# Retention in 64-token chunks with state and v stacked in K, the first layer run a block ahead, and weights split by layer

## The chip, the cores and the metric

The kernel runs on one core of a Trainium2 chip. The core has TensorE (PE) for matrix products, VectorE (DVE), ScalarE (ACT) and GpSimd (POOL) for elementwise work, and SyncE (SP), which here only starts transfers. The metric is the time of one execution on the device in microseconds (us), the median of several runs. Smaller is better. All arithmetic is in float32.

## The reference

Retention over 2 batches, 8 heads, 576 positions and head width 64 gives 1152 tokens of width 512. Four dense experts (512 to 1024 to 512, ReLU), weighted per token, follow; then one MLP (512 to 2048 to 512) with a mish-like activation.

```python
# retention
scores = (1 / sqrt(64)) * q @ k.T
Dmat = where(i >= j, gamma[h] ** (i - j), 0)
x = (scores * Dmat) @ v                     # then to [1152, 512]
# experts, e = 0..3
p = probs / (probs.sum(-1) + 1e-9)
out += p[:, e] * (relu(x @ w1[e]) @ w2[e])
# MLP
h = out @ w_in
y = (h * tanh(softplus(h))) @ w_out
```

## The kernel before, in words

**Retention.** The sequence of a batch is cut into 6 chunks of 96 tokens, 12 steps over both batches (loop `Fori(0, BATCH)`). For a step PE computes the masked scores of the next chunk (`scores`, L259, with q spread into a block-diagonal tile so that two heads share one product), the output from scores and v (L316), the output from the running state and q (L322), and the addition to the state k^T v (L296). ACT spreads q (L375) and copies the state out of PSUM (L387). DVE masks the scores (L480), scales the output with the decay of the rows (L510) and takes the low part of the split of x (L518). POOL scales v by the decay of the keys (L660).

**Splitting.** The large products use a fast format that keeps fewer bits, so each operand is kept as a high and a low part and each product is three matmuls: high by high (L265), high by low (L266), low by high (L267), each with 128 weights columns and 384 moving columns. ACT makes the high part of a weight (L186, `unit_hi`), POOL the low part (L191, `unit_lo`); for activations ACT makes `h_hi` (L416) and DVE `h_lo` (L525).

**Experts and MLP.** The MLP counts as two more "experts" of 1024 hidden columns. For each of 6 experts, 3 blocks of 384 tokens and 8 tiles of 128 hidden columns there are 12 matmuls of the first layer (`hidden`) and 12 of the second (`project`): 144 tiles, 3456 matmuls. The order on PE is written out by hand: the first layer of a tile is issued `AHEAD` = 3 tiles before its second layer. The hidden tiles go through a ring of `HR` = 4 PSUM banks, so a first layer also waits until the activation of four tiles earlier has been computed (`s_hf`). After each block DVE adds the four PSUM banks of the second layer to `acc_sb` (L546, L548). In the MLP each tile needs, one after the other, exp (ACT L438), `m_a` and `m_w` (DVE L596, L598), ln and exp (ACT L443, L445), `m_t` (POOL L686), `m_c`, `m_n`, `h_act` (DVE L605, L611, L614), then the split. Weights of an expert come in 8 units of 512 KB, each split in one operation of 128x1024 on ACT and one on POOL; the split of the next expert's units falls at the end of the last block of an expert and at the start of the next.

**Token weights.** DVE normalises the probabilities; ACT writes them to memory (`probs_by_expert<-p_norm`, L401), waits for that write (`s_ps`) at the last chunk of the first batch, and reads them back broadcast over the partitions (L407).

Of the kernel before, what the change touches and what calls it, by code (L numbers as in the profile page):

```python
# [19 lines left out]
CH = 96  # L36
CHUNKS = SEQ // CH
STEPS = BATCH * CHUNKS
PAIRS = HEADS // 2
MID = SEQ // 2  # L40
SLOTS = CHUNKS
# [6 lines left out]
TPE = PH * UNITS  # L48
KT = DM // P
UW = KT * P + DM  # L50
RAW = 4
HR = 4
AHEAD = 3
WARM = 9
LAG = 3

M0 = MOE_EXPERTS
# [3 lines left out]
def build(nc, qk_in, kv_in, row_decay_in, key_decay_in, mask_in, probs_in, weights_in, probs_dram, out_t):  # L62
    with ExitStack() as ctx:
# [3 lines left out]
        def sem(name):  # L67
            return ctx.enter_context(nc.semaphore(name))

        w_hi0 = sb("w_hi0", [P, RAW, UW], F32R)
        w_lo0 = sb("w_lo0", [P, RAW, UW], F32R)
        w_raw = sb("w_raw", [P, RAW, UW])
        x_hi = sb("x_hi", [P, KT, TOKENS], F32R)
        x_lo = sb("x_lo", [P, KT, TOKENS], F32R)
        acc_sb = sb("acc_sb", [P, KT, TOKENS])

        pb = sb("pb", [P, MOE_EXPERTS * TOKENS + TC])
# [9 lines left out]
        qk = sb("qk", [P, SLOTS, 2, PAIRS, CH], stack=attn)  # L89
        kv = sb("kv", [CH, SLOTS, 2, DM], stack=attn)  # L90
        row_decay = sb("row_decay", [P, CHUNKS, PAIRS, CH], stack=attn)
        key_decay = sb("key_decay", [CH, CHUNKS, HEADS], stack=attn)
        mask = sb("mask", [CH, CH], stack=attn)

        q_diag = sb("q_diag", [P, 2, PAIRS, 2, CH], stack=attn)
        s_masked = sb("s_masked", [CH, 2, PAIRS, 2, CH], stack=attn)

        state = sb("state", [P, 2, PAIRS, P], stack=attn)
# [3 lines left out]
        w_hi1 = sb("w_hi1", [P, UNITS - RAW, UW], F32R)  # L102
        w_lo1 = sb("w_lo1", [P, UNITS - RAW, UW], F32R)
        h_hi = sb("h_hi", [P, HR, TC], F32R)
        h_lo = sb("h_lo", [P, HR, TC], F32R)
        h_act = sb("h_act", [P, 2, TC])
# [7 lines left out]

        banks = [ctx.enter_context(nc.psum_tensor(f"bank{i}", [P, 512], F32)) for i in range(8)]

        HALF = PAIRS // 2
        ps_s = [[banks[2 * par + y][0:CH, 0:PAIRS * CH].rearrange("p (h x c) -> p h x c", h=HALF, x=2)
                 for y in range(2)] for par in range(2)]
        ps_state = banks[5][:, 0:PAIRS * DH].rearrange("p (h c) -> p h c", h=PAIRS)  # L120
        ps_o = [banks[6 + par][:, 0:PAIRS * CH].rearrange("p (h c) -> p h c", h=PAIRS) for par in range(2)]
        ps_acc = [banks[d][:, 0:TC] for d in range(KT)]
        ps_h = [banks[4 + i][:, 0:TC] for i in range(HR)]

        s_qk = [sem(f"s_qk{i}") for i in range(SLOTS)]
        s_kv = [sem(f"s_kv{i}") for i in range(SLOTS)]
        s_rowd = [sem(f"s_rowd{i}") for i in range(CHUNKS)]
        s_keyd = sem("s_keyd")
        s_mask = sem("s_mask")  # L130
        s_zs = sem("s_zs")
        s_qd = sem("s_qd")
# [3 lines left out]
        s_sm = sem("s_sm")  # L136
        s_o = sem("s_o")
        s_kvp = sem("s_kvp")
        s_st = sem("s_st")
# [6 lines left out]
        s_pb = sem("s_pb")  # L146
# [4 lines left out]
        s_g1 = sem("s_g1")  # L151
        s_acc = sem("s_acc")
        s_g2 = sem("s_g2")
# [51 lines left out]
        def _(sp):  # L205
# [547 lines left out]
```

## Time and profile before

| what | value |
|---|---|
| median of 3 runs | 688.27 us (685.68 to 689.82) |
| span of the profiled execution | 682.0 us |
| PE busy | 657.8 us (96%), 3993 matmuls |
| DVE busy | 362.5 us (53%) |
| ACT busy | 225.8 us (33%) |
| POOL busy | 187.2 us (27%) |
| memory traffic | 40.78 MB |

The span is the profiled execution from its first to its last instruction. No time of that execution as a whole is listed beside the span, so the 6.3 us between the span and the median of the runs are taken as what lies around the span. PE and PEld are the matmuls and the weight loads of TensorE; a matmul is pipelined with the next, so its own duration (some 337 ns) is longer than the distance to the next one. `L265` is line 265 of the kernel. The idle time in front of an instruction is named with what released it.

### The profile page before, as it was taken

Reading aid. Unit: us, or ns where it says so; the run is one execution under the profiler, and the core shown is the slowest. Engines: PE = TensorE matmul, PEld = TensorE weight load, DVE = VectorE, ACT = ScalarE, POOL = GpSimd, SP = SyncE. Lnnn points to the kernel's source line nnn. Section 1 sums busy time; section 2 is a strip of 40 time slices with the busy share of each in tenths; the row PEclk is TensorE's granted clock in tenths of the full one; section 3 lists DMA queues with packets and bytes.
Section 4 is the critical chain, followed back from the end, with each engine's and each line's share of the span. In section 5 each row is a group of like instructions: output and inputs, shape, how many; then the busy total and the mean of one; then the engine's idle time right before and its main releaser. Section 6 shows DMA issues by size and latency. Waiting matters only on the chain.

```text
span 682.0 us, 10838 instructions
## 1 busy us (share of the span) xinstructions
PE 657.8 (96%) x3993; PEld 643.8 (94%) x3993; DVE 362.5 (53%) x618; ACT 225.8 (33%) x405; POOL 187.2 (27%) x113
## 2 busy tenths in 40 slices
PE   8979999999999999999999999999899998799998
PEld 5868999999999999999999999999899997699997
DVE  5534532325232334232344242547997789988786
ACT  4554211133111133111133121235555454444442
POOL 2255400046000056000055000153423256532222
PEclk9989999999999999999999999999999999999999
DMA  9994300023000023000024000031100002001011
GB/s 276 293 281 167 123 1 1 1 93 124 31 0 0 0 92 134 20 0 0 0 93 153 0 0 0 0 122 63 62 0 0 0 31 92 0 0 46 0 46 46
DMA packets 13967, 40.78 MB, mean 60 GB/s; under 512 B 2304, under 2 KB 4608, under 8 KB 13952
## 3 DMA queue, kind: packets, MB, share of 16 engines
q1 hardware_dynamic: 12848, 38.22, 17.5%
q10 hardware_dynamic: 1104, 2.38, 1.1%
q8 instruction: 7, 0.11, 0.1%
q14 instruction: 8, 0.07, 0.0%
HBM read 38.22 MB, written 2.38 MB: 60 GB/s over the span
## 4 chain that ended last, share of the span: by engine, by line
PE 84%; DVE 7%; DMA 4%; ACT 2%; issue 2%; SPq 1%; DVEq 0%; ACTq 0%
PE bank L265 27%; PE bank L267 27%; PE bank L266 27%; DMA qk<-in_qk 4%; DVE m_a L596 3%; PE bank L259 1%; PE bank L322 1%; DVE m_c L605 1%; PE bank L316 1%; DVE m_w L598 1%; ACT m_u L438 1%; ACT w_hi L186 1%; DVE acc_sb L548 1%; ACT m_r L443 1%; DVE h_lo L525 1%
## 5 line engine op out<-in xcount | busy, mean ns | idle before, releaser
L265 PE MATMUL bank<-h_hi,w_hi 128*128 128x384 f32 x576 | 195.4, 339 | 12.9 <-DVE h_lo L525 11.3
L191 POOL TENSOR_TENSOR w_lo<-w_raw,w_hi 128x1024 fp32r<-128x1024 f32 x48 | 117.9, 2461 | 323.0 <-ACT w_hi L186 322.8
L266 PE MATMUL bank<-h_lo,w_hi 128*128 128x384 f32 x576 | 194.0, 337 | 0.0
L267 PE MATMUL bank<-h_hi,w_lo 128*128 128x384 f32 x576 | 194.0, 337 | 0.0
L267 PE MATMUL bank<-x_hi,w_lo 128*128 128x384 f32 x576 | 194.0, 337 | 0.0
L265 PE MATMUL bank<-x_hi,w_hi 128*128 128x384 f32 x576 | 193.7, 336 | 0.1
L266 PE MATMUL bank<-x_lo,w_hi 128*128 128x384 f32 x576 | 193.5, 336 | 0.0
L416 ACT ACTIVATE h_hi<-h_act 128x384 fp32r<-128x384 f32 x144 | 75.2, 522 | 290.2 <-DVE h_act L531 269.0
L531 DVE SCALAR_TENSOR_TENSOR h_act<-bank,pb 128x384 f32<-128x384 f32 x96 | 53.5, 557 | 178.8 <-PE bank L267 178.2
L525 DVE TENSOR_TENSOR h_lo<-h_act,h_hi 128x384 fp32r<-128x384 f32 x144 | 97.4, 676 | 67.2 <-ACT h_hi L416 67.2
L265 PEld LDWEIGHTS bank<-h_hi,w_hi 128*128 128x128 f32 x576 | 108.0, 187 | 16.9 <-DVE h_lo L525 13.8
L265 PEld LDWEIGHTS bank<-x_hi,w_hi 128*128 128x128 f32 x576 | 108.1, 188 | 0.3 <-issue 0.3
L266 PEld LDWEIGHTS bank<-x_lo,w_hi 128*128 128x128 f32 x576 | 108.2, 188 | 0.0
L266 PEld LDWEIGHTS bank<-h_lo,w_hi 128*128 128x128 f32 x576 | 108.1, 188 | 0.0
L267 PEld LDWEIGHTS bank<-x_hi,w_lo 128*128 128x128 f32 x576 | 108.1, 188 | 0.0
L267 PEld LDWEIGHTS bank<-h_hi,w_lo 128*128 128x128 f32 x576 | 108.0, 188 | 0.0
L686 POOL TENSOR_TENSOR m_t<-m_w,m_r 128x384 f32<-128x384 f32 x48 | 56.2, 1171 | 130.1 <-ACT m_r L445 130.1
L186 ACT ACTIVATE w_hi<-w_raw 128x1024 fp32r<-128x1024 f32 x48 | 50.7, 1056 | 34.3 <-PE bank L267 34.2
L596 DVE TENSOR_SCALAR m_a<-m_u 128x384 f32<-128x384 f32 x48 | 37.2, 775 | 29.8 <-ACT m_u L438 29.8
L443 ACT ACTIVATE m_r<-m_w 128x384 f32<-128x384 f32 x48 | 25.2, 526 | 46.6 <-DVE m_w L598 46.6
L438 ACT ACTIVATE m_u<-bank 128x384 f32<-128x384 f32 x48 | 23.3, 485 | 43.6 <-PE bank L267 43.6
L605 DVE SCALAR_TENSOR_TENSOR m_c<-m_r,m_t 128x384 f32<-128x384 f32 x48 | 30.7, 640 | 1.1 <-POOL m_t L686 0.3
(37 smaller groups left out, 321.3 us busy)
## 6 DMA issues: line engine op xcount, KB each, us to landing
w_raw<-in_weights SPq DMA_DIRECT2D x48, 512.0 KB, 3.3
qk<-in_qk SPq DMA_DIRECT2D x12, 384.0 KB, 13.3
kv<-in_kv SPq DMA_DIRECT2D x12, 384.0 KB, 14.6
pb<-probs_by_expert ACTq DMA_DIRECT2D x4, 576.0 KB, 8.9
out_t<-acc_sb SPq DMA_DIRECT2D x2, 768.0 KB, 3.6
row_decay<-in_row_decay SPq DMA_DIRECT2D x6, 192.0 KB, 7.6
out_t<-acc_sb SPq DMA_DIRECT2D x4, 192.0 KB, 1.9
mask<-in_mask SPq DMA_DIRECT2D x1, 36.0 KB, 3.7
```

The source lines that it names most:

```text
L186: act.activation(high(u), w_raw[:, u % RAW, :], ACT.Copy).then_inc(s_wh, 1)
L191: pool.tensor_tensor(low(u), w_raw[:, u % RAW, :], high(u).bitcast(F32), ALU.subtract).then_inc(s_wl, 1)
L265: pe.matmul(out, w[0], x[0], start=first, stop=False)
L266: pe.matmul(out, w[0], x[1], start=False, stop=False)
L267: return pe.matmul(out, w[1], x[0], start=False, stop=last)
L416: act.activation(h_hi[:, n % HR, :], h_act[:, n % 2, :], ACT.Copy).then_inc(s_hh, 1)
L443: act.activation(m_r[:, n % 2, :], m_w[:, n % 2, :], ACT.Ln, bias=2.0).then_inc(s_ln, 1)
L525: dve.tensor_tensor(h_lo[:, n % HR, :], h_act[:, n % 2, :], h_hi[:, n % HR, :].bitcast(F32), ALU.subtract).then_inc(s_hl, 1)
L531: dve.scalar_tensor_tensor(h_act[:, n % 2, :], ps_h[n % HR], 0.0, pb[:, bass.ds(e * TOKENS + (n // UNITS) * TC, TC)], ALU.max, ALU.mult).t ...
L596: dve.tensor_scalar(m_a[:, :], m_u[:, n % 2, :], MISH_CAP, 2.0, ALU.min, ALU.add).then_inc(s_ma, 1)
L605: dve.scalar_tensor_tensor(m_c[:, :], m_r[:, n % 2, :], 2.0, m_t[:, n % 2, :], ALU.mult, ALU.add).then_inc(s_mc, 1)
L686: pool.tensor_tensor(m_t[:, n % 2, :], m_w[:, n % 2, :], m_r[:, n % 2, :], ALU.mult)\
```

## The change

**Retention.** Chunks are of 64 tokens, 9 per batch, 18 in all. One tile `qkv` of 128 partitions holds a chunk: the lower 64 partitions ("keys") hold v and k by tokens, the upper 64 ("features") k and q by features. Scores of chunk c+1 read the upper half and write the lower half of PSUM; the state product of chunk c reads the lower half and writes the upper one; they alternate in PE's order (`scores_and_state`). ACT then copies the state over the k of the features half, and DVE writes the masked scores over the k of the keys half, so that `output` is one product of depth 128 per head, with v and the state stacked as weights and the masked scores and q stacked as moving operand. Spreading q (ACT L375), the state-by-q products (L322) and the two zeroed tiles go away. Row decays are made on DVE from a small constant tile in place of six loads.

**First layer ahead.** The first layer runs a block (8 tiles) ahead of the second, with `h_hi` and `h_lo` of 8 tiles each. The first 8 tiles of it are put in halves of 6 matmuls between the products of chunks 7 to 17. The PSUM ring of hidden tiles stays at 4.

**Weights.** A unit is split into two halves of 256 KB, one per layer; each is split by an operation of 128x512 (ACT, then POOL), spread over the blocks at 8 halves in 11 tiles by a table. There are 96 halves, of which 11 are split during retention.

**The MLP's second layer** has the tokens as weights columns and 512 moving columns of `w_hi`/`w_lo`: 9 matmuls of 128x512 for a tile in place of 12 of 128x384, into 3 PSUM banks, and the result is stored by tokens.

**Loops** are gone: every engine's program is written out, with constants in the waits. The read of the probabilities is issued on ACT at the start, the wait for `probs_by_expert` stands on ACT at chunk 2, and only 192 KB of the broadcast is read there.

```diff
-CH = 96
-CHUNKS = SEQ // CH
+CH = 64
+PER_BATCH = SEQ // CH
+CHUNKS = BATCH * PER_BATCH
...
+AFTER_SCORES = {7: (0, 0), 8: (1, 0), 9: (2, 0), 10: (3, 0), 11: (4, 0),
+                12: (5, 0), 13: (5, 1), 14: (6, 0), 15: (6, 1), 16: (7, 0), 17: (7, 1)}
+AFTER_OUTPUT = {7: (0, 1), 8: (1, 1), 9: (2, 1), 10: (3, 1), 11: (4, 1)}
...
+            def output(c):
...
+                for hp in range(PAIRS):
+                    for x in range(2):
+                        mm = pe.matmul(ps_o[DH * x:DH * (x + 1), hp], qkv[rows, c % SLOTS, 0, 2 * hp + x],
+                                       qkv[rows, c % SLOTS, 1, 2 * hp + x], start=True, stop=True)
...
+            for c in range(CHUNKS):
+                scores_and_state(c)
+                if c in AFTER_SCORES:
+                    hidden_half(*AFTER_SCORES[c])
+                output(c)
+                if c in AFTER_OUTPUT:
+                    hidden_half(*AFTER_OUTPUT[c])
+            for n in range(TILES):
+                if n + UNITS < TILES:
+                    hidden_ready(n + UNITS)
+                    hidden_products(n + UNITS, range(KT))
+                if n < MOE_TILES:
+                    project(n)
+                else:
+                    project_tokens(n)
...
+            def masked(c):
+
+                dve.wait_ge(s_sc, c + 1)
+                if has_state(c):
+                    dve.wait_ge(s_kv, states(c))
...
+                if c == 2:
+                    act.wait_ge(s_ps, 16)
+                    act.dma_start(pb[:, 0, 0:TC], probs_dram[0, 0:TC].partition_broadcast(P)).then_inc(s_pb0, 16)
```

How instructions stand on the engines: first PE in one step of the retention. Before, a step is state addition, scores of the next chunk, output from scores, output from the state (the names are PSUM banks, the tile of k and v, the spread q, the masked scores).

```order
L296 MATMUL bank<-kv 64x64 [waits s_st]
L296 MATMUL bank<-kv 64x64 x7
L255 REGISTER_ALU
L259 MATMUL bank<-q_diag,qk 96x192 [waits s_qd]
L259 MATMUL bank<-q_diag,qk 96x192 x3
L312 REGISTER_ALU
L316 MATMUL bank<-s_masked,kv 64x96 [waits s_sm]
L316 MATMUL bank<-s_masked,kv 64x96 x3
L316 MATMUL bank<-s_masked,kv 64x96 [waits s_sm]
L316 MATMUL bank<-s_masked,kv 64x96 x3
L322 MATMUL bank<-qk,state 128x96 x4
```

After, on PE at chunk 7: the last two of its 16 alternating score and state products, the first half of hidden tile 0, the 8 output products, and the start of that tile's second half.

```order
L268 MATMUL bank<-qkv 64x64
L272 MATMUL bank<-qkv 64x64
L314 MATMUL bank<-x_hi,w_hi 128x384 [waits s_wl,s_xl]
L315 MATMUL bank<-x_lo,w_hi 128x384
L316 MATMUL bank<-x_hi,w_lo 128x384
L314 MATMUL bank<-x_hi,w_hi 128x384
L315 MATMUL bank<-x_lo,w_hi 128x384
L316 MATMUL bank<-x_hi,w_lo 128x384
L308 MATMUL bank<-qkv 64x64 [waits s_st,s_xt,s_sm,s_vd]
L308 MATMUL bank<-qkv 64x64 x7
L314 MATMUL bank<-x_hi,w_hi 128x384
L315 MATMUL bank<-x_lo,w_hi 128x384
```

So the output products, which wait for the masked scores (`s_sm`), the copied state (`s_st`) and the row scaling of the chunk before (`s_xt`), stand right behind the scores and state products of the same chunk in chunks 0 to 6, and behind six first-layer matmuls from chunk 7 on.

ACT at the start of the changed kernel, from the state copy of chunk 0 to that of chunk 4:

```order
L409 ACTIVATE qkv<-bank 64x512 [waits s_kv,s_sc]
L445 DMA probs_by_expert<-p_norm 128x4x9 [waits s_pc]
L409 ACTIVATE qkv<-bank 64x512 [waits s_kv,s_sc]
L442 ACTIVATE x_hi<-x_tmp 128x4x64 [waits s_xt]
L409 ACTIVATE qkv<-bank 64x512 [waits s_kv,s_sc]
L442 ACTIVATE x_hi<-x_tmp 128x4x64 [waits s_xt]
L448 DMA pb<-probs_by_expert 128x384 [waits s_ps]
L409 ACTIVATE qkv<-bank 64x512 [waits s_kv,s_sc]
L442 ACTIVATE x_hi<-x_tmp 128x4x64 [waits s_xt]
L409 ACTIVATE qkv<-bank 64x512 [waits s_kv,s_sc]
```

The wait for the written probabilities (`s_ps`) has moved from the last chunk of the first batch to three state copies after the write is issued; the state copy of chunk 3 (the fourth L409 here) is queued behind it.

## Rows read from the trace of the kernel before

**Rows 1.** Page, parts 1 and 3: busy time by engine; instruction queues.

```profile
PE 657.8 (96%) x3993; PEld 643.8 (94%) x3993; DVE 362.5 (53%) x618; ACT 225.8 (33%) x405; POOL 187.2 (27%) x113
...
q8 instruction: 7, 0.11, 0.1%
```

**Rows 2.** Windows: start:end, length, busy us (instructions) by engine, PEclk, DMA share, GB/s.

```profile
10.00:20.00 10.00, 9.64 (x131) 8.26 (x130) 5.97 (x11) 5.70 (x13) 2.35 (x4) 1.00 1.05 306
...
36.00:40.00 4.00, 3.58 (x20) 2.87 (x22) 1.67 (x3) 2.59 (x5) 2.90 (x2) 0.57 1.03 270
...
100.00:450.00 350.00, 350.00 (x2003) 350.00 (x2002) 126.81 (x217) 75.66 (x118) 64.61 (x27) 1.00 0.11 39
450.00:500.00 50.00, 46.57 (x264) 45.46 (x262) 40.35 (x59) 23.74 (x44) 22.55 (x14) 1.00 0.19 63
550.00:600.00 50.00, 41.30 (x227) 39.07 (x227) 44.53 (x59) 24.84 (x45) 29.36 (x18) 1.00 0.13 42
```

**Rows 3.** Chain that ended last, 0 to 70 us: start, length, what.

```profile
4.96 5.79 DMA qk<-in_qk
...
30.38 21.28 DMA qk<-in_qk
...
67.56 0.44 PE bank L265
```

**Rows 4.** The same chain, MoE stage: one matmul of three blocks.

```profile
120.82 0.18 PE bank L265
...
221.58 0.18 PE bank L265
```

**Rows 5.** The same chain, one step of retention on PE.

```profile
19.26 0.62 PE bank L296 x16
19.88 1.47 PE bank L259 x8
21.35 0.81 PE bank L316 x16
22.16 1.06 PE bank L322 x8
```

**Rows 6.** Timeline, start of the kernel: start, length, engine, line, operation.

```profile
0.74 0.40 SPq L207 DMA_DIRECT2D qk<-in_qk  x1
...
7.59 1.07 ACT L375 ACTIVATE q_diag<-qk 64x384 f32<-64x384 f32 x2 [2.34 <-DMA qk<-in_qk]
```

**Rows 7.** DMA view: issuing engine, count, KB each, median us from issue to landing.

```profile
p_nat<-in_probs SPq DMA_DIRECT2D x1, 18.0 KB, 3.3
probs_by_expert<-p_norm ACTq DMA_DIRECT2D x1, 18.0 KB, 11.7
```

**Rows 8.** Groups by line: count, busy us, mean ns, idle before and releaser.

```profile
L387 ACT ACTIVATE state<-bank 64x256 f32<-64x256 f32 x20 | 7.6, 378 | 0.8 <-issue 0.2
L438 ACT ACTIVATE m_u<-bank 128x384 f32<-128x384 f32 x48 | 23.3, 485 | 43.6 <-PE bank L267 43.6
L480 DVE TENSOR_TENSOR s_masked<-bank,mask 96x384 f32<-96x384 f32 x24 | 12.4, 546 | 5.4 <-PE bank L259 5.3
L548 DVE TENSOR_TENSOR acc_sb<-bank,acc_sb 128x384 f32<-128x384 f32 x48 | 23.5, 549 | 0.9 <-PE bank L267 0.9
```

**Rows 9.** Timeline, PE after a wait in retention.

```profile
36.41 2.87 PE L259 MATMUL bank<-q_diag,qk 128*96 128x192 f32 x8 [2.28 <-ACT q_diag L375]
```

**Rows 10.** Timeline, MLP stage: DVE and POOL while weights are split.

```profile
565.70 2.39 POOL L191 TENSOR_TENSOR w_lo<-w_raw,w_hi 128x1024 fp32r<-128x1024 f32 x1
565.80 2.51 DVE L596 TENSOR_SCALAR m_a<-m_u 128x384 f32<-128x384 f32 x1 [0.34 <-ACT m_u L438]
571.37 2.38 DVE L596 TENSOR_SCALAR m_a<-m_u 128x384 f32<-128x384 f32 x1 [0.47 <-ACT m_u L438]
```

**Rows 11.** Timeline, MLP stage: DVE where no weights are split.

```profile
510.54 0.56 DVE L598 SCALAR_TENSOR_TENSOR m_w<-m_u,m_a 128x384 f32<-128x384 f32 x1
513.44 0.36 DVE L596 TENSOR_SCALAR m_a<-m_u 128x384 f32<-128x384 f32 x1 [0.22 <-ACT m_u L438]
513.84 0.56 DVE L598 SCALAR_TENSOR_TENSOR m_w<-m_u,m_a 128x384 f32<-128x384 f32 x1
```

**Rows 12.** Timeline, end: last matmul of PE.

```profile
678.68 0.34 PE L267 MATMUL bank<-h_hi,w_lo 128*128 128x384 f32 x1
```

**Rows 13.** Timeline, start of the second layer: PE's weight load.

```profile
67.55 0.19 PEld L265 LDWEIGHTS bank<-h_hi,w_hi 128*128 128x128 f32 x1 [1.05 <-issue]
```

More of the change, by code:

```diff
@@ new lines, in hidden_products, with hidden_half @@
+            def hidden_products(n, tiles):
+                c, t = n // UNITS % PH, n % UNITS
+                for k in tiles:
+                    at = slice(P * k, P * (k + 1))
+                    mm = three(ps_h[n % HR], (w_hi[:, 0, t, at], w_lo[:, 0, t, at]),
+                               (x_hi[:, k, cols(c)], x_lo[:, k, cols(c)]), k == 0, k == KT - 1)
+                if KT - 1 in tiles:
+                    mm.then_inc(s_g1, 1)
+            def hidden_half(t, half):
+                if half == 0:
+                    hidden_ready(t)
+                hidden_products(t, range(2 * half, 2 * half + 2))
@@ new lines, in project_tokens @@
+            def project_tokens(n):
+                g, t = n // UNITS, n % UNITS
+                if g % PH == 0:
+                    pe.wait_ge(s_wl, 2 * UNITS * (g // PH) + UNITS + t + 1)
+                pe.wait_ge(s_hl, n + 1)
+                for tt in range(TT):
+                    if t == 0:
+                        pe.wait_ge(s_af, emptied(g - 1, tt))
+                    rows = slice(P * tt, P * (tt + 1))
+                    mm = three(ps_out[tt], (h_hi[:, n % UNITS, rows], h_lo[:, n % UNITS, rows]),
+                               (w_hi[:, 1, t], w_lo[:, 1, t]), t == 0, t == UNITS - 1)
+                    if t == UNITS - 1 and tt < TT - 1:
+                        mm.then_inc(s_acc, 1)
+                mm.then_inc(s_g2, 1)
@@ L350, in _ @@
[L350 to L362 removed]
+            pe.wait_ge(s_slot[0], landed(0))
@@ new lines, in _ @@
+            for h in range(HEADS):
+                mm = scores_head(0, h)
+            mm.then_inc(s_sc, 1)
+            for c in range(CHUNKS):
[13 more added lines that the diff above has]
+                    project_tokens(n)
@@ L550, in add_up_from @@
-            def add_up_from(start, e, c):
-                with dve.If(e == start):
-                    add_up(e, c, first=True)
-                with dve.If(e > start):
-                    add_up(e, c)
-            def second_lo(c, tiles=range(KT)):
-                for d in tiles:
-                    dve.wait_ge(s_x2h, KT * c + d + 1)
-                    dve.tensor_tensor(x_lo[:, d, cols(c)], acc_sb[:, d, cols(c)],
-                                      x_hi[:, d, cols(c)].bitcast(F32), ALU.subtract)
```

836 lines of the change are left out of this document (381 added, 455 removed).

## The prediction, on record before the changed kernel ran

> **What bounds the kernel now.** I read the page first, then windows over the whole span, then the chain that ended last, and then timelines at the places where PE was not full. PE is busy 657.8 of 682.0 us [rows 1], and from 100 to 450 us it has no gap at all [rows 2]. There the kernel is a plain stream of matmuls. Its pace is read from the same place in blocks that are three apart: 221.58 - 120.82 = 100.76 us for 3 x 192 matmuls, 0.1749 us each [rows 4]. Of these, 160 ns are 384 columns at 2.4 GHz (granted clock 1.00) [rows 2]; 15 ns come on top.
>
> So the time of before divides into four pieces. Until 67.56 us runs the retention, with only 3 of the 144 first-layer tiles done; then the first second-layer matmul starts [rows 3]. The 3420 matmuls left take 3420 x 0.1749 = 598.3 us at that pace. The last matmul ends at 678.68 + 0.34 = 679.0 [rows 12], so 679.0 - 67.56 - 598.3 = 13.1 us are lost in between; 3.4 and 8.7 us of it are PE's idle time in 450 to 500 and 550 to 600 us [rows 2], both in the MLP, where DVE is busy 89% in the second. The last 3.0 us are the last addition and store.
>
> The retention is bound by input: transfers run at 306 GB/s with all 16 engines busy [rows 2], and the chain waits 5.8 and 21.3 us for q and k [rows 3]. One step costs PE 0.62 + 1.47 + 0.81 + 1.06 = 3.96 us [rows 5].
>
> **The change part by part.** *Retention on PE.* Each float32 product counts as two instructions. The nearest row for the new 64x64 products is L296, whose heads alternate between two halves of the output partitions: 16 in 0.62 us, 0.038 each [rows 5]. Scores and state together are 32 of them, 1.22 us; the output is 16, 0.61 us. That is 1.83 us for 64 tokens, 18 times 33 us, against 12 x 3.96 = 47.5 us. I take this, because scores and state alternate between disjoint halves too; the other bound is no overlap at all, 0.076 each.
>
> In chunks 0 to 6 nothing stands between the scores and the output. The output waits for the mask on DVE, which now also waits for the state product. L480 takes 0.546 us for 384 columns [rows 8], so 0.7 for 512; with 0.25 us of hand-over the chunk is 1.22 + 0.7 + 0.25 + 0.61 = 2.8 us. From chunk 7 on six first-layer matmuls (1.05 us) cover that chain, and they are work that would have to be done anyway.
>
> *Start.* Before, q of the second step was the seventh transfer, 1.45 MB in all, and was read at 7.59 us [rows 6]. Chunk 1 ends 1.27 MB (512 + 219 + 512 KB) after the same start, so about 7.0 us. Chunks 0 to 2 then end at 15.3, and the output of chunk 3 at 18.1.
>
> *The wait for the probabilities.* Their write took 11.7 us to land under full transfers, that of the read in the same state of the queues 3.3 [rows 7]. ACT issues it behind the state copy of chunk 0, which ends at 8.3 + 0.6 = 8.9 us (the copy by L387 and L438, 0.378 us for 256 columns and 0.485 for 384: 0.59 for 512 [rows 8]). It lands at 20.6. ACT has reached the wait at chunk 2 by about 15 us and stands there; behind it are the copy of the state of chunk 3 and every later x_hi. PE waits for that copy before the scores of chunk 4, from 18.1 to 20.6 + 0.3 (issue) + 0.6 (copy) + 0.2 = 21.7: 3.6 us. After such a wait of 2.3 us the granted clock was 0.57 for 4 us, half of it near the level of 1.2 GHz, and 8 instructions that take 1.47 us elsewhere took 2.87 [rows 2, 5, 9]: some 1.3 us more without the flight of the last one. The landing is bounded by 3.3 us (no wait, 4.9 us less) and by 11.7 x 4/3 = 15.6 us (packets of 4 KB ahead of it in place of 3 KB; 3.9 us more); I take the same instruction's own row.
>
> *Sum of the retention.* Chunks 4 to 6: 3 x 2.8 + 1.3, to 31.4. Chunks 7 to 11 with a whole hidden tile each: 1.22 + 0.61 + 2.10 = 3.93, 19.7 us, to 51.1. Chunks 12 to 16 with half a tile: 2.88, 14.4 us, to 65.5; chunk 17 1.7, to 67.2; joins 0.3: 67.5 us. That is where before stood too, but with 8 tiles done, not 3. Input is not the bound after chunk 7: 18 chunks, 8 halves and the small tiles are 11.9 MB, at 306 GB/s 39 us and a start of 2.
>
> *The stream after it.* 3456 - 96 = 3360 matmuls in the old count. Of them 576 (MLP, second layer) become 432 of 512 columns. The unknown is where the 15 ns on top go. If they are per matmul, one takes 213.3 + 15 = 228.3 ns; if in proportion to columns, 233.2. I take 228.3, since 15 ns a matmul is what the row shows beside the column time. 2784 x 0.1749 + 432 x 0.2283 = 486.9 + 98.6 = 585.5 us; the other bound gives 2.1 us more.
> Against this row stands a rule of the Trainium skill, TensorE: Matmul & The Clock Gate, section "Wait — 56ns, not 53.3ns?": only about 2.5 ns are added per warm matmul. By it 384 columns would take 162.5 ns and not the 174.9 measured, so this trace doesn't agree; with 215.8 ns the 432 would be 93.2 us, 5.4 less.
>
> *The MLP.* Now the 12 us. While POOL runs `w_lo` for 2.39 us, DVE's `m_a`, 0.36 us elsewhere, takes 2.51 us and ends with it; a tile then costs DVE 571.37 - 565.80 = 5.57 us [rows 10, 11]. PE needs 4.15 to 4.2. Without a split a tile costs DVE 513.84 - 510.54 - 0.22 = 3.08 us [rows 11]. With a half (1.2 us of POOL) I count 5.57 - 1.2 = 4.37. Additions are 3 a block, 0.549 x 512/384 = 0.73 each [rows 8]. From PE's tile 105 to 125 there are 16 halves: 16 x 4.37 + 5 x 3.08 + 2 x 2.2 = 89.7 against 21 x 4.15 = 87.2; from 88 to 101 (10 halves, 2 additions, 8 splits of the second x at 0.55) 64.8 against 58. DVE may fall some 6 us behind before PE waits, because the hidden tile that needs its bank stands four tiles on. So it is nearly hidden: I allow 4 us of the 13.1. If that cover is gone, all 13.1 come back.
>
> *End.* The last addition has a third more columns (0.2 us), the last matmul likewise: 3.4 us for 3.0.
>
> *No loops.* PE's program grows from 759 to 3612 rows. I cost it at nothing: the packets of its instruction queue took 0.1% of the transfer engines' time [rows 1], and PE executes about as many matmuls as before.
>
> **Sum:** 67.5 + 585.5 + 4.0 + 3.4 = 660.4 us for a span of 682.0. The span of before lies 6.3 us under the median; carried over, 666.7, say 667 us, 3% faster. Of the 21.6 us, 12.7 are the first-layer tiles done earlier (5 x 12 x 0.1749 = 10.5) and the wider matmuls (2.2), 9 the stalls of the MLP.
>
> **The rivals.** *The write lands early.* No wait on ACT at chunk 2; for it speaks the 3.3 us of the read, against it that the row of 11.7 is the same instruction: 667 - 4.9 = 662.
> *Wide matmuls run at the column rate.* 512 columns in 213.3 ns, all else as before: 432 x 15 ns = 6.5 us less, 660. Against it speaks the 174.9 of the stream. The rule named above is this rival in a weaker form.
> *DVE becomes the bound in the MLP.* Several small splits, each meeting the next tile's `m_a` or `m_n`, leave no tile at 3.08; for it speaks DVE's 89% where PE waited [rows 2], against it the shorter POOL operation. 13.1 in place of 4: 676.
> *Scores and state don't overlap.* They use disjoint rows and columns of the array and read other partitions than L296 does; at 0.076 each, 16 chunks cost 1.22 more: 19.5 us, 686, no change.
> *The written-out program is fetched too slowly.* This one ends slower. 7 packets of 0.11 MB served 759 rows [rows 1]; 3612 rows need 34. Where PE entered its loop over the experts its weight load waited 1.05 us for nothing the profile shows [rows 13]. At that price, 27 more refills cost 28 us: 695. It decides from 0.95 us a refill; below 0.8 the kernel stays faster.
> A rule speaks against this rival: the Trainium skill, Runtime: NRT & Kernel Launch, section "Instruction fetch mechanics", says that a program streams in blocks of 16 KiB with the next one fetched ahead, and that taken branches are what costs. No row here shows the fetch itself.
>
> **How the numbers follow.** My forecast (663 to 671) 0.45; write early 0.13; wide matmuls at the column rate 0.10; DVE bound 0.18; no overlap 0.06; fetch 0.04; something faster than all of these 0.04. The range takes in the first four, 0.86, from 656 (early write and cheap matmuls together: 667 - 4.9 - 6.5) to 679 (DVE bound and a late write in part). About 0.5% is what a measurement of this kernel can tell from no change. Faster by more than that (under 684.8) has 0.90, the same 0.06, slower 0.04.
>
> **What would show it.** Right: a wait of ACT for `probs_by_expert` of some 5 us near 15 to 21 us, and of PE of 3 to 4 behind it; the state and score instructions at 0.038 us; the first second-layer matmul between 68 and 71 us; 100% PE through the MoE stage at 33.6 us a block; projections of the MLP at 0.228 us; PE idle under 6 us in the MLP. Wrong: PE's sequencer named as what is waited for, `m_a` above 1.2 us on average, chunks 7 to 11 longer than 4.2 us, or PE idle without a name at even distances.

## The result and the profile after

| kernel | median of the runs | runs | span of the profiled run |
|---|---|---|---|
| before | 686.97 us (684.88 to 689.82) | 4 | 682.0 us |
| after | 656.00 us (655.74 to 660.01) | 4 | 653.9 us |

The ratio is 0.9537, with a 95% interval of 0.9486 to 0.9589: 4.6% faster, where 3% was forecast (667 us). The median lies on the lower end of the range (656). The profiled run itself took 655.74 us, 1.8 us more than its span. Here and below a median is that of all runs of a comparison, while ratio and interval leave out runs more than 1.5% above the fastest of their kernel.

The page of the changed kernel, parts 1 and 3, to be set against [rows 1]:

```profile
PE 638.8 (98%) x4153; PEld 609.8 (93%) x4153; DVE 357.3 (55%) x624; ACT 219.7 (34%) x431; POOL 204.4 (31%) x167
...
q8 instruction: 33, 0.54, 0.3%
```

PE is full for 98% of a span that is 28 us shorter. The instruction queue moved 33 packets (the prediction counted 34). Writing the loops out cost no time, as `before_unrolled` below shows.

Windows of the changed kernel (start:end, length, busy us and instructions by engine, granted clock, DMA share, GB/s; the engines are PE, PEld, DVE, ACT, POOL in this order), against [rows 2]:

```profile
10.00:20.00 10.00, 6.22 (x171) 5.52 (x167) 6.52 (x14) 3.45 (x7) 5.35 (x5) 1.00 1.05 405
100.00:450.00 350.00, 350.00 (x2021) 350.00 (x2020) 122.80 (x225) 82.95 (x158) 76.22 (x60) 1.00 0.15 43
450.00:500.00 50.00, 50.00 (x265) 46.86 (x264) 48.42 (x79) 27.95 (x58) 24.57 (x20) 1.00 0.14 43
500.00:550.00 50.00, 48.90 (x245) 43.87 (x244) 48.74 (x78) 27.66 (x56) 24.86 (x21) 1.00 0.15 43
550.00:600.00 50.00, 50.00 (x252) 45.34 (x251) 48.42 (x79) 28.36 (x58) 26.00 (x21) 1.00 0.00 1
```

Two things are to be seen. In the same 350 us of the MoE stage, without a gap in either kernel, PE starts 2021 matmuls and not 2003: the pace itself has changed, from 174.9 to 173.3 ns. And in the MLP PE is idle 1.1 us from 450 to 600 us, where it was idle 3.4 and 8.7, although DVE is busy 97% of each window.

The chain that ended last, in retention, at the start of the stream, and at the longest of the two stops of the MLP:

```profile
1.65 5.40 DMA qkv<-in_chunks
...
8.40 8.72 DMA probs_by_expert<-p_norm
17.14 0.34 ACTq L448
17.59 0.60 ACT qkv L409
...
26.69 1.28 POOL w_lo L218
...
28.11 0.41 PE bank L314
...
501.07 0.61 DVE acc_sb L540
501.68 0.14 issue
501.82 0.47 PE bank L314
```

Timeline of ACT at its wait for the probabilities, and of PE at the output of chunks 3, 4 and 5 (start, length, and in brackets the idle time in front and its releaser):

```profile
17.59 0.59 ACT L409 ACTIVATE qkv<-bank 64x512 f32<-64x512 f32 x1 [2.90 <-DMA probs_by_expert<-p_norm]
```

```profile
17.14 0.69 PE L308 MATMUL bank<-qkv 128*64 128x64 f32 x16 [0.93 <-issue]
20.37 0.69 PE L308 MATMUL bank<-qkv 128*64 128x64 f32 x16 [0.90 <-DVE qkv L479]
23.06 0.69 PE L308 MATMUL bank<-qkv 128*64 128x64 f32 x16 [0.93 <-issue]
```

The write was issued at 8.40 and landed 8.7 us later, not 11.7. ACT stood for 2.9 us. A chunk without hidden work then takes 23.06 - 20.37 = 2.69 us; the one behind the wait took 20.37 - 17.14 = 3.23, so PE lost 0.5 us by it.

Timeline of PE where the stream begins, against the last row of [rows 3]:

```profile
65.37 0.44 PE L314 MATMUL bank<-x_hi,w_hi 128*128 128x384 f32 x1
...
67.62 0.41 PE L314 MATMUL bank<-h_hi,w_hi 128*128 128x384 f32 x1
```

The first second-layer matmul starts at 67.62 in place of 67.56 us, with 9 first-layer tiles done. The kernel before had done 4 by then, so 5 x 12 = 60 matmuls or 10.4 us are gained there.

DVE and POOL of the changed kernel in the MLP (groups by line, and one timeline), against [rows 10, 11]:

```profile
L558 DVE SCALAR_TENSOR_TENSOR m_w<-m_u,m_a 128x384 f32<-128x384 f32 x48 | 42.4, 882 | 1.7
L556 DVE TENSOR_SCALAR m_a<-m_u 128x384 f32<-128x384 f32 x48 | 24.7, 515 | 13.8 <-ACT m_u L428 13.8
```

```profile
562.06 1.40 POOL L218 TENSOR_TENSOR w_lo<-w_raw,w_hi 128x512 fp32r<-128x512 f32 x1
```

```profile
562.35 1.53 DVE L558 SCALAR_TENSOR_TENSOR m_w<-m_u,m_a 128x384 f32<-128x384 f32 x1
566.53 0.56 DVE L558 SCALAR_TENSOR_TENSOR m_w<-m_u,m_a 128x384 f32<-128x384 f32 x1
```

The effect of [rows 10] is still there: `m_w`, 0.56 us when POOL is free, takes 1.53 us and ends 0.4 us behind `w_lo`. Where a split meets DVE it costs about 1 us now (1.53 - 0.56); `m_a` lost 2.15 us before (2.51 - 0.36).

### The profile page after: what moved, and what is told of

The parts are those of the page before. It is cut to its first block, busy times and chain, and to the rows that moved or that the text cites. A ratio compares the mean times of both kernels' runs of the same rounds, so it can differ in the third digit from the quotient of the medians.

```text
span 653.9 us, 10358 instructions
## 1 busy us (share of the span) xinstructions
PE 638.8 (98%) x4153; PEld 609.8 (93%) x4153; DVE 357.3 (55%) x624; ACT 219.7 (34%) x431; POOL 204.4 (31%) x167
## 4 chain that ended last, share of the span: by engine, by line
PE 85%; DVE 9%; DMA 2%; issue 2%; ACT 1%; POOL 0%; SPq 0%; ACTq 0%; DVEq 0%
PE bank L314 28%; PE bank L316 27%; PE bank L315 27%; DVE m_n L568 2%; PE bank L268 2%; DVE m_a L556 1%; DVE m_w L558 1%; DMA probs_by_expert<-p_norm 1%; PE bank L308 1%; DVE m_c L565 1%; DVE h_lo L500 1%; DMA qkv<-in_chunks 1%; DVE x_lo L547 1%; DVE acc_sb L542 0%; ACT qkv L409 0%
## 5 line engine op out<-in xcount | busy, mean ns | idle before, releaser
L218 POOL TENSOR_TENSOR w_lo<-w_raw,w_hi 128x512 fp32r<-128x512 f32 x96 | 129.5, 1350 | 305.1 <-ACT w_hi L212 305.1
L314 PE MATMUL bank<-h_hi,w_hi 128*128 128x384 f32 x384 | 128.3, 334 | 0.0
L315 PE MATMUL bank<-h_lo,w_hi 128*128 128x384 f32 x384 | 128.3, 334 | 0.0
L316 PE MATMUL bank<-h_hi,w_lo 128*128 128x384 f32 x384 | 128.3, 334 | 0.0
L315 PEld LDWEIGHTS bank<-h_lo,w_hi 128*128 128x128 f32 x384 | 72.1, 188 | 0.0
L212 ACT ACTIVATE w_hi<-w_raw 128x512 fp32r<-128x512 f32 x96 | 59.1, 618 | 17.8 <-PE bank L316 17.8
L314 PE MATMUL bank<-w_hi,h_hi 128*128 128x512 f32 x144 | 56.2, 390 | 1.3 <-DVE acc_sb L540 1.1
L316 PE MATMUL bank<-w_hi,h_lo 128*128 128x512 f32 x144 | 56.8, 395 | 0.0
L315 PE MATMUL bank<-w_lo,h_hi 128*128 128x512 f32 x144 | 56.7, 394 | 0.0
L558 DVE SCALAR_TENSOR_TENSOR m_w<-m_u,m_a 128x384 f32<-128x384 f32 x48 | 42.4, 882 | 1.7
```

Of the source, the lines that this page charges most:

```text
L212: act.activation(w_hi[:, part, u], w_raw[:, half % RAW], ACT.Copy).then_inc(s_wh, 1)
L218: pool.tensor_tensor(w_lo[:, part, u], w_raw[:, half % RAW], w_hi[:, part, u].bitcast(F32), ALU.subtract).then_inc(s_wl, 1)
L314: pe.matmul(out, w[0], x[0], start=first, stop=False)
L315: pe.matmul(out, w[0], x[1], start=False, stop=False)
L316: return pe.matmul(out, w[1], x[0], start=False, stop=last)
L558: dve.scalar_tensor_tensor(m_w[:, n % 2, :], m_u[:, n % 2, :], MISH_CAP, m_a[:, :], ALU.min, ALU.mult).then_inc(s_w, 1)
```

## The experiments

**The MLP's stalls: are they POOL's long splits?** Three edits of the kernel before and one of the changed kernel.

`before_short`. Leaves out most of the low parts of the weights in the MLP:

```diff
-                pool.tensor_tensor(low(u), w_raw[:, u % RAW, :], high(u).bitcast(F32),
+                pool.tensor_tensor(low(u)[:, 0:8], w_raw[:, u % RAW, 0:8], high(u)[:, 0:8].bitcast(F32),
```

> The kernel before with POOL's low part of the weights cut to 8 of 1024 columns while the MLP runs (those weights are not split, the rest is as before). Theory A (DVE waits for POOL's operation of 2.4 us, and PE for DVE): m_a falls to 0.36 to 0.45 us on average, the MLP's stalls of PE from 13 to 15 us to under 3, the span is 11 to 13 us shorter. Theory B (three tiles of lead are too little for the chain exp, w, r, t, c, n whatever POOL does): stalls of over 8 us stay.

672.18 us (667.48 to 677.52, 4 runs), ratio 0.9731 [0.9672, 0.9789]. From 450 to 500 and from 550 to 600 us:

```profile
450.00:500.00 50.00, 50.00 (x288) 50.00 (x287) 36.14 (x61) 26.22 (x48) 19.30 (x15) 1.00 0.26 84
550.00:600.00 50.00, 50.00 (x288) 50.00 (x287) 37.10 (x76) 30.64 (x56) 15.53 (x20) 1.00 0.13 42
```

The stops of [rows 2] are gone, all 13.8 us of them (the distances between PE's starts in the MLP, each less the usual one, added up). POOL's part of the splits makes them.

`before_quarters`. The same work in shorter operations, back to back:

```diff
-            pool.tensor_tensor(low(u), w_raw[:, u % RAW, :], high(u).bitcast(F32),
-                               ALU.subtract).then_inc(s_wl, 1)
+            for at in range(0, UW, UW // 4):
+                part = slice(at, at + UW // 4)
+                lo = pool.tensor_tensor(low(u)[:, part], w_raw[:, u % RAW, part], high(u)[:, part].bitcast(F32),
+                                        ALU.subtract)
+            lo.then_inc(s_wl, 1)
```

> The kernel before with each low part of the weights made by four POOL operations of 256 columns one behind the other, in place of one of 1024. Theory A (DVE waits for the operation that is running, so its length counts): m_a waits for one quarter at most, its longest falls from 2.5 to about 1.0 us, and the stalls of the MLP to under 7 us, the span 6 to 10 us shorter. Theory B (it is POOL's total time that counts, since POOL goes from one operation to the next without letting DVE in): m_a stays at up to 2.5 us and the span within 2 us, or longer by POOL's fixed cost.

679.71 us (678.12 to 685.06, 10 runs), ratio 0.9897 [0.9868, 0.9926]. Stops of 8.7 us stay of 13.8. The groups by line show where: `m_a` is cheap again (398 ns, 775 before), but `m_w` is slower (664 ns, 558 before). That it meets the next quarter is the likely reading.

```profile
L599 DVE TENSOR_SCALAR m_a<-m_u 128x384 f32<-128x384 f32 x48 | 19.1, 398 | 29.5 <-ACT m_u L441 29.5
L601 DVE SCALAR_TENSOR_TENSOR m_w<-m_u,m_a 128x384 f32<-128x384 f32 x48 | 31.9, 664 | 1.7
```

`after_short`. The same omission in the changed kernel, `w_lo` of 8 of 512 columns in the MLP.

> The changed kernel with POOL's low part of the weights cut to 8 of 512 columns from the first mish tile on (those weights are not split). Theory A (DVE waits for POOL, and the 2.0 us of PE's two stalls in the MLP and the uneven matmul distances of 229 to 236 and 175 to 185 ns both follow from PE meeting DVE's results late): stalls 0, distances 173.3 and 226.7 throughout, span 4 to 5 us shorter. Theory B (the uneven distances are PE's own): stalls 0, distances stay, 2 us shorter.

656.95 us (654.47 to 657.59, 4 runs), ratio 0.9551 [0.9487, 0.9614]; PE's stops fall from 2.0 to 0.6 us. There was no more to be had here. The uneven distances of the MLP (see the wide matmuls below) stay. The times say nothing: the retention of the profiled run had 10.2 us at the 1.2 GHz level, and three of the four runs have a mean clock of 0.992 to 0.995.

`after_look4`. Is it the split or the longer lookahead that removed the stops? The first layer only 4 tiles ahead (the kernel before has 3):

```diff
+LOOK = 4
...
-        after = 1 + 11 * k // 8 if k < UNITS else 12 + 11 * (k - UNITS) // 8
+        after = 5 + k if k < UNITS else 13 + 11 * (k - UNITS) // 8
...
-                if n + UNITS < TILES:
-                    hidden_ready(n + UNITS)
-                    hidden_products(n + UNITS, range(KT))
+                if n + LOOK < TILES:
+                    hidden_ready(n + LOOK)
+                    hidden_products(n + LOOK, range(KT))
```

> The changed kernel with its first layer 4 tiles ahead instead of 8, as in the kernel before: in retention only tiles 0 to 3 are begun, in halves in chunks 10 to 17, and the splits of first-layer weights are moved 4 tiles later to fit; splits stay 512 columns wide. Theory W (the short lookahead makes the uneven distances of the kernel before): mean distance of 100 to 450 us 174.9 instead of 173.3 ns. Theory O: 173.3 ns stays. On the stalls of the last stage: if the lookahead of 8 tiles is what removed them, PE waits 8 to 14 us again after 460 us; if the narrower splits did (the theory so far), it waits 2 to 4 us. Retention and stream together should cost what they cost in the changed kernel when the clock stays up (656 to 662 us in all); each stretch of low clock as in the run with no first-layer tile in retention would add 5 us or more.

663.44 us (661.99 to 665.32, 4 runs), ratio 0.9646 [0.9558, 0.9734]. From 450 to 600 us, this kernel:

```profile
450.00:600.00 150.00, 148.68 (x758) 135.60 (x757) 135.41 (x223) 82.45 (x168) 72.55 (x58) 1.00 0.11 31
```

and the changed kernel:

```profile
450.00:600.00 150.00, 148.90 (x759) 136.07 (x758) 145.58 (x234) 83.98 (x172) 75.44 (x60) 1.00 0.10 29
```

1.3 us idle against 1.1: it was the narrower, spread-out splits that removed the stops, not the step from 4 to 8 tiles ahead. A lookahead of 3 with these splits was not run, and narrow and spread out were not taken apart in the changed kernel. The 7 us come from retention, below.

**The retention: what do the first-layer tiles in it bring?** `after_noahead` runs the first 8 tiles behind the last chunk:

```diff
-                if c in AFTER_SCORES:
-                    hidden_half(*AFTER_SCORES[c])
                 output(c)
-                if c in AFTER_OUTPUT:
-                    hidden_half(*AFTER_OUTPUT[c])
+            for t in range(UNITS):
+                hidden_half(t, 0)
+                hidden_half(t, 1)
```

> The changed kernel with the 16 halves of the first layer behind the retention and not in it; the same work otherwise. Theory A (they cover the chain from the scores over the mask to the output, some 0.9 us a chunk): each of chunks 7 to 17 costs 2.7 us alone, so 5 x (2.7 + 2.1 - 4.2) + 6 x (2.7 + 1.05 - 2.95) = 7.8 us more, less the 1.1 us of the wait at chunk 12: the span is 6 to 8 us longer than that of the changed kernel. Theory B (they are the same PE work in another place): within 2 us of it.

670.27 us (669.0 to 674.1, 4 runs), ratio 0.9763 [0.971, 0.9815]: 14 us lost, twice what was expected. Windows of the stretch before the clock first falls, and of the two stretches in which it is low (the clock is the number behind POOL's count):

```profile
8.00:18.70 10.70, 6.22 (x173) 5.68 (x175) 6.73 (x14) 3.62 (x7) 6.45 (x6) 1.00 1.04 404
18.70:32.30 13.60, 10.37 (x170) 9.36 (x165) 6.62 (x15) 4.42 (x9) 2.67 (x3) 0.50 0.77 283
39.20:52.80 13.60, 10.78 (x175) 9.76 (x171) 5.07 (x11) 4.69 (x10) 9.05 (x9) 0.50 0.63 205
```

The granted clock stood at 1.2 GHz for 27 us in all, and a chunk cost 3.95 us there in place of 2.69. That is some 7 chunks of 1.26 us, about 9 us. The other 6 to 7 us of the 15.4 between the two spans (669.3 and 653.9) are the lost cover, as expected.

Did the tiles keep the clock up? The mean granted clock over the span was 0.980 to 0.990 in all four runs of this kernel, and 1.0 (0.999 or more) in 7 of 8 runs of the changed one. So low stretches are rarer with the tiles. But the first stretch can't be laid to missing tiles: it begins at 18.7 us, and up to there both kernels run the same instructions on PE, since the first tile comes at 28.1. The changed kernel in the same window, with its clock up:

```profile
8.00:18.70 10.70, 6.44 (x183) 5.76 (x179) 6.70 (x14) 3.62 (x7) 6.88 (x7) 1.00 1.05 408
```

Only the second stretch lies where the tiles stand. What they do for the clock is thus likely, not shown. `after_look4`, which begins four tiles in chunks 10 to 17 only, has 0.989 to 0.992 in its four runs and 0.86 from 35 to 70 us of its profile:

```profile
35.00:70.00 35.00, 31.57 (x485) 28.04 (x486) 22.26 (x42) 16.01 (x32) 21.34 (x19) 0.86 0.55 178
```

35 us at 0.86 are some 10 us at half clock, which would slow PE's work there by 5 us. Most of the rest is earlier: the outputs of its chunks 1 to 3 are 3.95 us apart, as at the low level. The clock does not hold in every run with the tiles either: one of the changed kernel (660.01 us) has 0.989, `after_short` lost it for 10.2 us, and three of six runs of `after_both` below have 0.987 to 0.994. Nor is every long run one of low clock: a run of 659.62 us (`after_repeat`) has 1.0, and what made it longer is open.

**The two waits left in retention.** `after_both`:

```diff
-                if c == 2:
+                if c == 4:
                     act.wait_ge(s_ps, 16)
...
                 pool.wait_ge(s_slot[c % SLOTS], landed(c))
+                if c > 12:
+                    pool.wait_ge(s_xl, c - 2)
```

> The changed kernel with ACT's wait for the written probabilities at chunk 4 in place of chunk 2, and POOL's scaling of v for chunks 13 to 17 held back until the low part of x of two chunks earlier is made. By the trace of the changed kernel the state copy of chunk 3 then starts at 16.35 in place of 17.59 us (1.2 us), and the 1.07 us wait at chunk 12 goes: span 1.8 to 2.3 us shorter than 653.9. Rival: chunk 7 gets its weights no sooner, so the first 1.2 us reappear as a wait there: 0.8 to 1.1 us.

Its profiled run had a span of 651.9 us, 2.0 under that of the changed kernel. Its chain has the outputs of chunks 1, 2 and 4:

```profile
11.19 0.69 PE bank L308 x16
13.88 0.69 PE bank L308 x16
19.26 0.69 PE bank L308 x16
```

Chunks 2 and 4 are twice 2.69 us apart, so the wait for the write had cost PE the 0.5 us read above, not the 1.2 expected here. The pacing of POOL gave 0.8: the output of chunk 14 comes 2.94 us behind that of chunk 13, and came 3.74 behind it (53.20 and 56.94). Another 0.6 us is no gain of the edits: the output of chunk 1 stands at 11.19 for 11.76, ahead of both. The median over 6 runs is 656.62 us (653.77 to 659.94), ratio 0.9563 [0.9511, 0.9614], not to be told from the changed kernel's. `after_repeat`, the changed kernel once more on the same chip, gave 656.21 us (656.04 to 659.62, 4 runs), ratio 0.9568 [0.9503, 0.9632].

> The changed kernel again, to stand beside its variants on the same chip. Span 653.5 to 654.5 and a time 1.8 us above it; the kernel before has a span of 682 to 688 us from run to run, also about 2 us under its time. If the kernel before has a steady span of 682 and a time 6 us above it, my step from span to time was right and the changed kernel's was another.

**The wide matmuls of the MLP.** `after_narrow` has 12 of 128x384 again, stored by features:

```diff
-                if n < MOE_TILES:
-                    project(n)
-                else:
-                    project_tokens(n)
+                project(n)
```

> The changed kernel with the MLP's second layer as before, 12 matmuls of 128x384 a tile with the weights stationary, four banks, output transposed. Theory A (a matmul costs its columns plus 32 cycles, 13.3 ns): 576 x 173.3 = 99.8 against 432 x 226.7 = 97.9 us, so 1.9 us longer, and the extra 67 ns a tile that the MLP shows beside these two go or stay. Theory B (the cost is in proportion to columns, what is seen comes from elsewhere): within 0.5 us of the changed kernel.

655.88 us (654.48 to 658.74, 4 runs), ratio 0.9561 [0.9497, 0.9625]. The span is 652.7, and 0.4 of the 1.2 us under the changed kernel's stand ahead of the second layer (it starts at 67.22 for 67.62). So the wide form brings nothing. Timeline of PE in the changed kernel, last of the 9 wide ones and the first hidden ones:

```profile
566.52 0.39 PE L316 MATMUL bank<-w_hi,h_lo 128*128 128x512 f32 x1
566.75 0.33 PE L314 MATMUL bank<-x_hi,w_hi 128*128 128x384 f32 x1
566.92 0.34 PE L315 MATMUL bank<-x_lo,w_hi 128*128 128x384 f32 x1
567.09 0.34 PE L316 MATMUL bank<-x_hi,w_lo 128*128 128x384 f32 x1
567.27 0.35 PE L314 MATMUL bank<-x_hi,w_hi 128*128 128x384 f32 x1
567.46 0.34 PE L315 MATMUL bank<-x_lo,w_hi 128*128 128x384 f32 x1
...
568.85 0.39 PE L314 MATMUL bank<-w_hi,h_hi 128*128 128x512 f32 x1
```

The distances between starts are uneven, up to 0.19 behind the wide ones, and a wide one takes 0.23 (568.85 - 566.75 = 2.10 us for 12 hidden ones, where 12 x 0.1733 is 2.08). At the very end, where wide ones stand alone, they take 226.7 ns each.
**Where does the pace of 174.9 ns come from?** The forecast carried it over, and it is 173.3 now. `before_unrolled` writes the kernel before without loops:

```diff
-            with pe.Fori(0, EXPERTS) as e:
+            for e in range(0, EXPERTS):
```

> The kernel before with every loop and branch written out and constants in its waits, nothing else changed. Theory A (the 1.6 ns by which a matmul of the stream costs more before, 174.9 against 173.3 ns, come from the loops' registers and branches): the stream falls to 33.28 us per 192 matmuls, the 1.05 us at the start of the second layer go, and the span is 6 to 7 us shorter. Theory B (they come from where the weights and activations lie, or from how near the first layer is to the second): the block stays at 33.59 us and the span moves by less than 2 us. The stalls in the MLP stay at 13 to 15 us in both.

687.67 us (683.56 to 693.74, 12 runs), ratio 1.0025 [0.9993, 1.0058]. Theory B holds: the windows below show the same pace, though the instruction queue moved 31 packets for the 7 of [rows 1]. Then the layout of the weights, in both directions: `after_units` and `before_layers`.

```diff
-        w_hi = sb("w_hi", [P, 2, UNITS, DM], F32R)
+        w_hi0 = sb("w_hi0", [P, RAW // 2, 2, DM], F32R)
+        w_hi1 = sb("w_hi1", [P, UNITS - RAW // 2, 2, DM], F32R)
```

```diff
-        w_hi0 = sb("w_hi0", [P, RAW, UW], F32R)
+        w_hi0 = sb("w_hi0", [P, 2, RAW, DM], F32R)
```

> The changed kernel with only its weight storage put back as in the kernel before: two pairs of tensors for units 0 to 3 and 4 to 7, both layers of a unit side by side. Order, waits and sizes of all instructions stay. Theory L (the layout makes the short uneven distances): the mean distance of first- and second-layer matmuls in the stretch 100 to 450 us goes from 173.3 to 174.9 ns, with distances of 171, 175, 178, 185 ns appearing; 2784 matmuls times 1.6 ns is 4.4 us more, so about 660.5 us where the changed kernel takes 656. Theory O (the order of matmuls and the length of the lookahead make them): distances stay at 173.3 ns and the time at 656.

656.25 us (656.03 to 656.58, 4 runs), ratio 0.9543 [0.9502, 0.9584].

> The kernel before with only its weight storage changed: in each of the two pairs of tensors the first-layer halves of four units stand together, then the second-layer halves, as the changed kernel does for eight. Theory L: the mean distance of 100 to 450 us falls from 174.9 to near 173.3 ns, 4 to 5 us less, ratio about 0.993. Theory O: 174.9 ns stays and the time is that of the kernel before, ratio 1.00.

687.77 us (684.52 to 690.93, 10 runs), ratio 0.9991 [0.9958, 1.0025]. Then the place in SBUF, `before_low`:

```diff
         w_lo0 = sb("w_lo0", [P, RAW, UW], F32R)
+        w_hi1 = sb("w_hi1", [P, UNITS - RAW, UW], F32R)
+        w_lo1 = sb("w_lo1", [P, UNITS - RAW, UW], F32R)
         w_raw = sb("w_raw", [P, RAW, UW])
...
-        w_hi1 = sb("w_hi1", [P, UNITS - RAW, UW], F32R)
-        w_lo1 = sb("w_lo1", [P, UNITS - RAW, UW], F32R)
+        acc_sb = sb("acc_sb", [P, KT, TOKENS])
```

> The kernel before with only places in SBUF exchanged: the weight tensors of units 4 to 7 move down, next to those of units 0 to 3, and the sums over experts (acc_sb) move up into the place that they had. Instructions, order and waits stay. Theory P (a tensor's place in SBUF makes the uneven distances): the mean distance of 100 to 450 us falls from 174.9 towards 173.3 ns, up to 4.5 us less, ratio about 0.993. Theory O (the order of the matmuls and of what the other engines do meanwhile): 174.9 ns stays, ratio 1.00.

682.69 us (679.43 to 689.86, 10 runs), ratio 0.9939 [0.9903, 0.9975]. The windows of 100 to 450 us of `before_unrolled`, `before_layers`, `before_low`, `after_units` and `after_look4`, in this order:

```profile
100.00:450.00 350.00, 350.00 (x2003) 350.00 (x2002) 128.88 (x216) 75.63 (x118) 64.93 (x27) 1.00 0.12 40
```

```profile
100.00:450.00 350.00, 350.00 (x2003) 350.00 (x2002) 128.26 (x219) 75.13 (x119) 63.59 (x26) 1.00 0.11 38
```

```profile
100.00:450.00 350.00, 350.00 (x2018) 350.00 (x2017) 128.47 (x221) 76.12 (x119) 64.52 (x27) 1.00 0.12 39
```

```profile
100.00:450.00 350.00, 350.00 (x2020) 350.00 (x2019) 122.60 (x225) 82.89 (x158) 76.62 (x60) 1.00 0.14 43
```

```profile
100.00:450.00 350.00, 350.00 (x2021) 350.00 (x2020) 140.29 (x216) 76.66 (x147) 73.66 (x56) 1.00 0.14 42
```

Loops, layout and lookahead leave the count of matmuls where it was (2003; 2020 and 2021). Exchanging places alone moves it from 2003 to 2018: 1.3 ns a matmul, and 4.4 us over the 3408. Theory P holds for 1.3 of the 1.6 ns. Which address counts, and for which operand, stays open: by the exchange `w_raw`, `x_hi` and `x_lo` move too, and `after_units` has two of its four weight tensors in a high place and yet 2020 matmuls (173.5 ns each). The obvious guess was that loaded weights from high places are slow, in the MLP's wide form too, where `h_hi` and `h_lo` are the loaded side. `after_hlow` moves them down:

```diff
-        w_raw = sb("w_raw", [P, RAW, DM])
+        h_hi = sb("h_hi", [P, UNITS, TC], F32R)
+        h_lo = sb("h_lo", [P, UNITS, TC], F32R)
```

> The changed kernel with places in SBUF exchanged alone: h_hi and h_lo stand right above the weights, w_raw moves up above the probabilities. Theory P2 (weights that PE loads from the upper part of SBUF make the distances uneven, in the kernel before w_hi1 and w_lo1, in the last stage of the changed one h_hi and h_lo, which are the loaded side there): the uneven distances of the last stage go away, 67 ns a tile, 2.7 us less: span 651.3, time 653. Theory Q (the 512 columns of that stage make them, the place mattered only in the kernel before): distances and time stay, 656.

> The same exchange of places, with the two edits in retention (the probabilities' write awaited at chunk 4, v-decays from chunk 13 paced), last stage in 512 columns. Theory P2: 651.9 less 2.7, span 649.2, time 651.0, that is 1.9 us under the version with 12 narrow products (652.9), the saving that the wide form was to bring. Theory Q: 652 to 654, not under the narrow version.

655.78 us (655.66 to 659.66, 6 runs), ratio 0.9546 [0.951, 0.9582], and the distances of the MLP stay as uneven. `after_best`: 655.33 us (653.71 to 658.81, 6 runs), ratio 0.9538 [0.9499, 0.9577]. The guess falls. The uneven distances of the MLP go with the wide form (`after_narrow` has none), and why is open.

**The best version.** `after_all` is `after_both` with the narrow products of `after_narrow`.

> The changed kernel with the three edits that each took something off a span: the wait for the probabilities' write at chunk 4 instead of 2, the v-decays from chunk 13 paced with the chunks, and the last layer's products in 12 matmuls of 128x384 instead of 9 of 512 columns. If the gains add (1.2 and 1.1 us in retention, 1.3 us in the last stage) the span is 650.5 us and the time 652.3. If they hide each other, the span stays at 652 and the time at 654 to 656.

652.91 us (652.73 to 653.31, 6 runs), ratio 0.9495 [0.9464, 0.9526], span 650.9. The gains add (0.7 of the 3.0 us of span stand ahead of the edits, chunk 1 at 11.08 for 11.76), and it was the fastest of all. Two versions with the same edits in retention but wide matmuls spread from 653.7 to 659.9; that this one doesn't isn't explained.

## Why the prediction was right in direction and short in size

The profiled run stands 11.0 us under the 666.7 of the sum (655.7). By its steps:

- **What lies around the span** is the step that failed most clearly: "The span of before lies 6.3 us under the median; carried over". It is 1.7 to 1.9 us in every run of either kernel (up to 2.2 in a variant, `before_quarters`):

```text
after        655.74 us, span 653.9      after_all    652.73 us, span 650.9
before       684.24 us, span 682.4      before       687.71 us, span 685.9
```

(`after_all` is the best version; the two lower ones are the kernel before again.) The other 4.5 us were the spread of the kernel before, whose runs reach from 682.1 to 694.0 us over all comparisons. Its profiled span of 682.0 was one of its shortest executions. A span must be set against its own run's time; where that isn't listed, the difference to a median of another execution isn't a constant to carry. This is 4.5 of the 11 us. In return the stated gain (21.6 us of span) has to be compared with 28.1 of span and 31 of median. The 3 us between these two are not traced; the clock may be in them. Over all comparisons 16 runs of the kernel before at a mean clock of 0.997 took 684.6 us on average, and 7 at 0.988 took 690.1.
- **The wait for the probabilities** was mis-sized. The place, the engine and what stood behind it were right, but the landing took 8.7 us and not 11.7, and PE lost 0.5 us and not 3.6. No low clock followed: the 1.3 us for it were 0. That is 4.4 us too much.
- **Chunks.** 2.69 us for 2.8. With a whole tile 4.19 and not 3.93, with half a tile 2.94 and not 2.88; and 0.8 us of a burst of v-decays on POOL before the output at 56.94, which I had not seen. The retention ended at 65.4 for 67.5. That its sum is off by 2.1 only is in part luck: it was 4.9 us too long up to chunk 6 and 2.8 too short from chunk 7 on. The overlap of scores and state is there: 32 in 1.0 us, under the 1.22 taken from L296.
- **The stream.** 2784 x 0.1733 = 482.5 us, 4.4 less than at 0.1749. I read that pace as a property of the matmul; `before_low` shows most of it, 1.3 of 1.6 ns, as one of where the tensors of the kernel before lay. The rule that I weighed against it (the Trainium skill, TensorE: Matmul & The Clock Gate, section "Wait — 56ns, not 53.3ns?": 2.5 ns a matmul on top) agrees no better: the even distances are 13.3 ns over the column time at 384 and at 512 columns.
- **The wide matmuls.** All else apart, they took 585.3 - 482.5 - 2.0 = 100.8 us for 98.6, with the uneven neighbours in it. In their place 576 narrow ones would take 99.8. So the 2.2 us of gain that I gave them are none.
- **The stalls of the MLP.** 4 allowed, 2.0 measured; before they were 13.8 (the gaps themselves; I had 13.1 by subtraction, with 3 tiles done where the rows give 4, 48 matmuls before 67.56: that would have been 15.4, the uneven distances of the MLP among it). The mechanism, DVE held up while POOL splits, was right. The cover that I named, the bank that is needed again four tiles on, is untested: no run has another ring than four banks.
- **End.** 3.2 us for 3.4, from the last matmul's end at 650.7. **No loops**: nothing, as costed; the rival of the slow fetch is refuted by `before_unrolled`.

Sum in the span: -2.1 (retention), -4.2 (stream and stalls), -0.2 (end) make 653.9 of 660.4. Of the 11.0 us, 4.5 are thus the carried difference, 4.4 the wait, 4.4 the pace and 2.0 the stalls; too little was put down for chunks 7 to 16 (2.8) and for the wide matmuls (2.2), and the rest is small. The mechanisms were right and these sizes off. Of the rivals, the early write came near in its price (4.4 of its 4.9 us) and less so in its landing (8.7 us, where it put 3.3). "Wide matmuls at the column rate", with all else as before, did not happen. The low end of the range, 656, was built from these two together; that the measured time stands there is luck in so far as other terms brought it there.

The 28.1 us of span come to: first-layer tiles run earlier, 60 x 0.1754 = 10.5 (0.1754 is (679.0 - 67.56 - 13.8) / 3408, the mean before); stalls of the MLP 13.8 - 2.0 = 11.8; the pace of the other 3348, the wide form included, 587.2 - (650.7 - 67.62 - 2.0) = 6.1; less 0.3 at the start and the end. Shown by experiments are the splits as the cause of the stalls, the cover of the tiles in retention, and the exchange of places as a cause of the pace in the kernel before. That the changed kernel owes its 173.3 ns to its places alone was not shown.

## What to carry to other kernels

Before a pace between matmuls goes into a sum, look at whether the distances are even. Where they aren't, other places in SBUF for the operands are worth a try: one exchange gave 1.3 ns a matmul here, another (`after_hlow`) nothing. Where such GpSimd and VectorE operations share a stage, count a meeting as a delay of VectorE of most of the GpSimd operation's length (2.15 us under one of 2.39, 0.97 under one of 1.40), and make them short and far apart; four short ones in a row recovered only 5 of 13.8 us. Set a profiled span against the time of its own run. Work that fills PE's waits may earn more than the wait it fills, since low clock was rarer with it.

## What was not expected of the hardware

- The same instructions in the same order run at 174.9 or 173.6 ns a matmul, by where tensors lie in SBUF (`before_low`).
- After the same work (PE busy 6.2 and 6.4 of 10.7 us), the granted clock fell to 1.2 GHz at 18.7 us in one kernel and stayed at 2.4 in the other (`after_noahead` and the changed kernel).
- 9 matmuls of 512 columns between 12 of 384 took longer (4.187 us a tile) than 24 of 384 (4.160).
- A small write of 18 KB landed after 11.7 us under transfers of 306 GB/s, and after 8.7 us under 405 GB/s.
